# U's six transfers on ScalarE's queue, separate signals for U's lower parts, and K's maximum subtracted in two instructions

## What is computed

```python
def phi(x):                                   # 128 features, then both signs: 256
    proj = einsum('bhsd,df->bhsf', x, w_phi)
    proj = proj - max(abs(proj), axis=-1)
    return concatenate([exp(proj), exp(-proj)])
q_p, k_p = phi(q), phi(k)
kv  = einsum('bhsf,bhsd->bhfd', k_p, v);  z = sum(k_p, tokens)
x   = (q_p @ kv) / (q_p @ z + 1e-6)           # heads side by side: 576 x 512
h   = x.T @ U @ V;  u = x + h.T               # U: 576 x 32, V: 32 x 576
x2  = u + relu(u @ w_ch1) @ w_ch2             # 512 -> 2048 -> 512
h   = relu(x2.T @ w_tok1) @ w_tok2;  u = x2 + h.T
out = u + relu(u @ w2_ch1) @ w2_ch2           # 512 -> 1536 -> 512
```

## Time and profile before

| | us |
|---|---|
| median of 3 runs (lowest, highest) | 965.28 (965.09, 967.3) |
| profiled execution, its own time | 961.59 |
| its span | 959.6 |
| PE busy | 953.0, 99% |
| PE weight loads (PEld) | 828.7, 86% |
| DVE busy | 510.3, 53% |
| ACT busy | 373.4, 39% |
| POOL busy | 238.1, 25% |

### The profile page before, as it was taken

One profiled execution on the slowest core, in us unless ns is written; L12 is line 12 of the kernel. 1 busy time (PEld: TensorE's weight loads), 2 busy tenths in 40 slices (PEclk: granted clock), 3 DMA queues, 4 the chain that ended last, 5 costly groups with the idle time before them and its releaser, 6 DMA issues.

```text
span 959.6 us, 14152 instructions
## 1 busy us (share of the span) xinstructions
PE 953.0 (99%) x5398; PEld 828.7 (86%) x5398; DVE 510.3 (53%) x1005; ACT 373.4 (39%) x795; POOL 238.1 (25%) x148
## 2 busy tenths in 40 slices
PE   8999999999999999999999999999999999999998
PEld 7998888888888888888888889988888888888898
DVE  6756777667777658777542332433443343343232
ACT  6757667726675445665321112322202211111111
POOL 4357566704344214432120002530000000000000
PEclk9999999999999999999999999999999999999999
DMA  7651111111111011110052005532142132010010
GB/s 194 179 206 29 45 29 37 44 44 44 30 37 44 22 59 29 45 44 9 7 182 89 23 1 176 182 99 77 50 116 83 50 94 92 13 44 1 1 44 23
DMA packets 43043, 62.75 MB, mean 65 GB/s; under 512 B 10657, under 2 KB 30305, under 8 KB 41953
## 3 DMA queue, kind: packets, MB, share of 16 engines
q1 hardware_dynamic: 34752, 52.59, 18.0%
q10 hardware_dynamic: 8224, 9.26, 2.9%
HBM read 47.68 MB, written 14.16 MB: 64 GB/s over the span
## 4 chain that ended last, share of the span: by engine, by line
PE 97%; SPq 1%; DMA 1%; DVE 1%; issue 0%; ACT 0%; ACTq 0%; DVEq 0%
PE ps_ring L875 50%; PE ps_a L875 15%; PE ps_m L875 8%; PE ps_m L748 5%; PE ps_t L719 2%; PE ps_ring L757 1%; PE ps_a L775 1%; PE ps_a L770 1%; PE ps_a L769 1%; PE ps_a L710 1%; PE ps_t L732 1%; PE ps_t L661 1%; PE ps_t L660 1%; PE ps_t L659 1%; PE ps_m L743 1%; PE ps_a L788 1%
## 5 line engine op out<-in xcount | busy, mean ns | idle before, releaser
L875 PE MATMUL ps_ring<-u_hi,w_hi 128*128 128x512 f32 (+1 forms) x376 | 143.5, 382 | 0.1
L875 PE MATMUL ps_ring<-h_hi,w_hi 128*128 128x512 f32 (+1 forms) x376 | 143.0, 380 | 0.0
L875 PE MATMUL ps_ring<-u_hi,w_lo 128*128 128x512 f32 (+1 forms) x376 | 141.0, 375 | 0.0
L875 PE MATMUL ps_ring<-u_lo,w_hi 128*128 128x512 f32 (+1 forms) x376 | 140.9, 375 | 0.0
L875 PE MATMUL ps_ring<-h_lo,w_hi 128*128 128x512 f32 (+1 forms) x376 | 140.8, 374 | 0.0
L875 PE MATMUL ps_ring<-h_hi,w_lo 128*128 128x512 f32 (+1 forms) x376 | 140.5, 374 | 0.0
L1028 ACT ACTIVATE h_hi<-ps_ring 128x512 fp32r<-128x512 f32 (+1 forms) x94 | 53.1, 565 | 173.9 <-PE ps_ring L875 173.2
L1255 DVE SCALAR_TENSOR_TENSOR h_lo<-ps_ring,h_hi 128x512 fp32r<-128x512 f32 (+1 forms) x94 | 60.8, 649 | 106.6 <-ACT h_hi L1028 106.5
L1320 POOL TENSOR_TENSOR q_features_lo<-q_features_t,q_features_hi 128x576 fp32r<-128x576 f32 x48 | 67.7, 1432 | 116.9 <-ACT q_features_t L957 116.9
L1338 POOL TENSOR_TENSOR w_lo<-w_raw,w_hi 128x1024 fp32r<-128x1024 f32 x28 | 67.6, 2430 | 116.6 <-ACT w_hi L988 115.4
L875 PEld LDWEIGHTS ps_ring<-h_lo,w_hi 128*128 128x128 f32 x376 | 70.8, 188 | 13.4 <-DVE h_lo L1255 0.2
(11 more groups left out here) (218 smaller groups left out, 1948.2 us busy)
## 6 DMA issues: line engine op xcount, KB each, us to landing
w_raw<-in_wa SPq DMA_DIRECT2D x16, 512.0 KB, 5.0
w_raw<-in_wb SPq DMA_DIRECT2D x12, 512.0 KB, 3.9
v_one<-in_v_aug SPq DMA_DIRECT2D x28, 165.0 KB, 2.2
x_features<-x_scratch SPq DMA_DIRECT2D x4, 1152.0 KB, 5.9
x_by_tokens<-x_turned SPq DMA_DIRECT2D x16, 288.0 KB, 5.4
u_full<-x_scratch SPq DMA_DIRECT2D x4, 1152.0 KB, 5.1
kq_raw<-in_q_t SPq DMA_DIRECT2D x28, 160.0 KB, 2.9
x_tokens<-x_by_tokens SPq DMA_DIRECT2D x16, 256.0 KB, 2.7
```

The source lines that it names most:

```text
L875: last = pe.matmul(ps, w, x, start=(k, m) == (0, 0), stop=ended)
```

## The change

Four edits.

1. U's six transfers are taken out of SyncE's list and issued by ScalarE, two each ahead of `kv(0)`, `exp_k(1)` and `kv(1)` in its list: the four full tiles, the upper half, the lower half of the last.
2. `diff_last`, a new signal: in batch 0 VectorE subtracts the maximum in two instructions, first the last tile (128x128), then the four full ones (128x512). The exp of the last tile waits for the first, the other two for the second.
3. `xl_done` is raised by both instructions of VectorE's `pair_t`. `pair_l` waits for the first ahead of its first matmul and for the second ahead of its fifth. The other waits for `xl_done` count double.
4. `WARM[1]` is 5 for 3.

```diff
-WARM = 10, 3
+WARM = 10, 5
...
-            if n == 2:
-                for cols in (slice(0, RANK), slice(2 * RANK, P)):
-                    sp.dma_start(U4[:, 0:FULL, cols], u4[:, 0:FULL, cols]).then_inc(sem["u4_in"], 16)
-                    for rows in HALF:
-                        sp.dma_start(U4[rows, FULL, cols], u4[HALF[0], FULL, cols]).then_inc(sem["u4_in"], 16)
...
-                    pe.wait_ge(sem["xl_done"], (B - 1) * DT)
+                    pe.wait_ge(sem["xl_done"], 2 * (B - 1) * DT)
...
-            wait(pe, "xl_done", pairs - DT)
+            wait(pe, "xl_done", 2 * (pairs - DT))
...
-                pe.wait_ge(sem["xl_done"], pn - DT + 1)
+                pe.wait_ge(sem["xl_done"], 2 * (pn - DT) + 1)
                 for t in range(ST):
+                    if t == FULL:
+                        pe.wait_ge(sem["xl_done"], 2 * (pn - DT) + 2)
...
-                act.wait_ge(sem["diff_done"], n + 1)
+                act.wait_ge(sem["diff_last" if first else "diff_done"], n + 1)
...
                     act.activation(kp(n)[:, 2 * FULL], DIFF0[:, FULL], ACT.Exp, scale=SIGN[:])
+                    act.wait_ge(sem["diff_done"], n + 1)
...
+        def load_u4(rows, tiles, source):
+            for cols in (slice(0, RANK), slice(2 * RANK, P)):
+                act.dma_start(U4[rows, tiles, cols], u4[source, tiles, cols]).then_inc(sem["u4_in"], 16)
+
         for name, n in PROLOGUE["act"]:
+            if (name, n) == ("kv", 0):
+                load_u4(slice(0, P), slice(0, FULL), slice(0, P))
+            if (name, n) == ("exp_k", 1):
+                load_u4(HALF[0], FULL, HALF[0])
+            if (name, n) == ("kv", 1):
+                load_u4(HALF[1], FULL, HALF[0])
...
-                    dve.tensor_tensor(DIFF0[:], proj, MK[:, 0:ST].unsqueeze(2).to_broadcast([P, ST, DF]),
-                                      ALU.subtract).then_inc(sem["diff_done"], 1)
+
+                    for tiles, done in ((slice(FULL, ST), "diff_last"), (slice(0, FULL), "diff_done")):
+                        dve.tensor_tensor(DIFF0[:, tiles], proj[:, tiles], MK[:, tiles].unsqueeze(2).to_broadcast(
+                            [P, tiles.stop - tiles.start, DF]), ALU.subtract).then_inc(sem[done], 1)
...
-                                  XPH[:, 0:FULL].rearrange("p t f -> p (t f)").bitcast(F32), ALU.subtract)
+                                  XPH[:, 0:FULL].rearrange("p t f -> p (t f)").bitcast(F32), ALU.subtract).then_inc(sem["xl_done"], 1)
```

More of the change, by code:

```diff
@@ L502, in mixer_kernel @@
         rk_in_0 rk_in_1 rk_again_0 rk_again_1 rq_in_0 rq_in_1 v_in_0 v_in_1 k0_hi k0_lo k_split_hi k_split_lo q_split_hi q_split_lo
-        pk_done tsum_done mk_done diff_done kp_done pqt_done rq_done mt_done mrow_done mhi_done mlo_done mt_spread
+        pk_done tsum_done mk_done diff_last diff_done kp_done pqt_done rq_done mt_done mrow_done mhi_done mlo_done mt_spread
         pt_done qp_done qpl_done v_ones kv_done kv_copied kvl_done out_done den_turned den_done rden_done rden_rows x_done
```

## The result

The changed kernel takes **959.44 us** (959.08 to 960.68, 4 executions). Beside it, on the same chip, the kernel before took 966.29 us (965.09, 965.28, 967.3, 968.15). The ratio is 0.993, 95% interval 0.9908 to 0.9951, so 6.9 us less. The profiled execution took 959.12 us, its span is 957.1 (961.59 and 959.6 before). Between the two profiled executions the gain is thus only 2.5 us, close to the 2.8 of the forecast. The other 4.4 are the subject of this text.

The account below looks back on a forecast made before the run. TensorE, busy 953.0 of 959.6 us, was taken as the bound, with gains at kv(2) and the 12 pair_l steps: 0.80 + 1.98 = 2.8 us off the median 965.28 gave 962.5 us, range 960.4 to 965.5.

Parts of the forecast that it names:

- The step that failed: Final sum: the 2.8 us gain on the profiled execution was applied to the runs' median, 965.28, giving 962.5.
- The forecast's own upper bounds: Largest gains allowed: 0.95 us at kv(2) and 2.85 us at the pair_l steps.
- U's transfers off SyncE's queue: Head 4's K issued near 13.7 instead of 16.68, so kv(2) loses its wait; 0.80 us (0.55 to 0.95).
- The rival that the transfers are the bound: Head 4's K still lands at 21.9 and kv(2) stays; 963.3 us, chance 0.08.
- The six issues on ScalarE: U's issues in ScalarE's program, 1.2 to 1.7 us per two, covered by its idle times; cost taken as 0.
- The slower rival: ScalarE stands still while issuing, 1.64 us for each of six; 4.0 us slower, 969.3 us, chance 0.06.
- Two subtractions: Batch 0 on VectorE: 0.08 us more per head, four-tile exps 0.24 sooner; sum 0 within 0.1 outside kv(2).
- Warm-ups: Four added passes, some 0.5 us, fill part of the 0.8 us before turn_r(0); worth 0.
- The pairs: Two signals at pair_l: 0.27 us at three long sites, 0.13 at nine short ones; 1.98 us together.
- the first rival: The pairs give their gain back, as TensorE then waits for ScalarE or VectorE; 964.5 us, chance 0.12.
- the rival by which all the weight loads' idle time comes back: At pair_l all the idle time returns, 2.85 us, 3.7 us in all; 961.6 us, chance 0.14.
- What is released behind L811 starts from TensorE's ends and moves with them: Argument that work behind pair_l's product moves earlier with TensorE, so the pairs' gain is not given back.

Follow-up runs that it names:

- warm5_only: Kernel before with only the warm-up calls ahead of turn_r(0) raised from three to five; 963.01 us, ratio 0.9994.
- pairs_only: Kernel before with only the two signals for U's lower parts at pair_l; 964.89 us, ratio 0.9987.
- diff_only: Kernel before with only the subtraction split in two; 966.92 us, ratio 1.001.
- u_only: Kernel before with only U's six transfers moved to ScalarE's queue; 961.22 us, ratio 0.9957.
- u_later_sp: Kernel before with U's six transfers still on SyncE's queue, but behind head 4's K; 961.00 us, ratio 0.9959.
- u_diff: Kernel before with U's transfers on ScalarE's queue and the two subtractions; 960.89 us, ratio 0.9951.
- u_pairs: Kernel before with U's transfers on ScalarE's queue and the two signals for U's lower parts; 960.26 us, ratio 0.9946.
- after_warm3: Changed kernel with the warm-up calls ahead of turn_r(0) back at three; 959.61 us, ratio 0.9956.
- after_swap: Changed kernel with VectorE's turn_r(1) put ahead of its out(0); 959.46 us, ratio 0.9939.
- fill_kv2: Kernel before with four more calls of products on ones on TensorE ahead of kv(2); 962.35 us, ratio 0.9979.
- six_small_sp: Kernel before with U's transfers on ScalarE's queue and six 16-row by 8-column transfers at their old place on SyncE's; 961.85 us, ratio 0.9973.

## Why the prediction was wrong, point by point

**The step that failed** is one sentence: "the median of the runs, 965.28, lies 3.7 above, and the same gain there gives 962.5". It took the 3.7 us between the profiled execution and the median for a constant. It is not: it is what the fall of the clock costs in the executions that have one, and the change takes away what led to it. At clock 1.0 the kernel before takes 961.9 and the changed one 959.6, 2.3 less; the rest of the 5.8 to 6.9 us is that two thirds of the old executions were longer, most by 3 to 7 us, and none of the new ones is. The range failed by the same step: the scatter of the runs before, 965.09 to 967.3, was read as noise about a median. The profiled execution itself took 961.59; three executions of 965.09 or more beside it say that something in them is different which the one profile does not hold. (The forecast's own upper bounds, 0.95 and 2.85, add to 3.8, not 3.7; nothing hangs on it.)

How sure the cause is: with head 4's K late, the clock stood in 47 of 139 executions (before, warm5_only, pairs_only, diff_only); with K early in 83 of 87 (u_only, u_later_sp, u_diff, u_pairs, after_warm3, and the changed kernel and after_swap, 16 and 12); with K late and four calls run in the wait in 11 of 12. Both profiles that caught a fall show it inside the idle time at kv(2). That idle time there leads to the fall is shown. What decides it in a single execution is open, and the length of the idle time alone does not: there was no fall with 0.70 us at kv(2) (the profile before) nor with 0.98 (fill_kv2), one with 1.67 and one with 1.17, but that one came when only 0.4 us of it had passed; and none with 1.17 us ahead of turn_r(0) in u_only. Four executions in 87 fell with K early, one of them only to 0.998 and 961.37 us. No profile shows one of these, nor one of the twelve at 970 to 978 before; a late K of a later head, as in u_pairs, is a possible cause, not a shown one.

**U's transfers off SyncE's queue: right.** K of head 3 at 9.56 (9.6 foretold), of head 4 at 13.57 (13.7), its copy at 20.00 (20.23), kv(2) at 22.67 for 22.8 to 23.0, directly behind turn_r(2). It stands 1.03 sooner, for 0.80. The two traces must be read from the same place, though: kv(0) is already 0.16 sooner, and turn_r(0) lies anywhere from 9.27 (pairs_only) to 9.79 (diff_only), and at 10.85 in warm5_only. From kv(0) to kv(2) it is 14.05 us before, 13.24 in u_only and 13.18 in the changed kernel, so U's move is worth 0.81 there. The rival that the transfers are the bound is refuted by this, and six_small_sp shows the issues at work.

**The six issues on ScalarE: right, 0.** They took 0.39, 0.53, 0.47, 0.61 and 1.12 for two, 3.1 us for 3.6 to 5.0 foretold, and run beside its casts and exps: the copy (L919) starts at 9.62 while the first issue lasts until 9.67. v_k's copy is at 11.72. The slower rival is gone with it.

**Two subtractions: right in mechanism.** From the first's start to the block maximum it is 0.81 (20.81 to 21.62) for 0.74 before, 0.07 more, so the second is not held, as by the rule of the Trainium skill (VectorE: DVE Perf Modes, Two Vector instructions with no wait between them). The forecast put their worth at 0 outside kv(2). From head 0's first subtraction to kv(0) it is 1.85 us in u_diff and 1.93 in u_only and before, and from kv(0) to kv(3) 21.12 for 21.25: 0.2 us in all, of which 0.06 falls between kv(0) and kv(2). The 0.41 between the two kernels' times has scatter in it; u_diff is already 0.35 ahead at turn_r(0).

**Warm-ups: right, 0.**

**The pairs: 1.98 foretold, 1.33 measured**, and here the first rival was half right. The lead of the changed kernel over the one before, read at equal instructions of the two traces, is 1.13 us ahead of the first pair (101 us) and 2.46 behind the last (474 us), and stays there to the end. At the sites themselves it rises by 0.13 to 0.16 at the nine short ones and 0.29 to 0.30 at the three long ones, 2.2 in all, more than foretold, though less than the 2.85 of the rival by which all the weight loads' idle time comes back. But 0.8 to 0.9 of this is given back within some us. Behind the fourth pair (long) and the eighth (long), PEld before, then after:

```profile
201.40 0.19 PEld L829 LDWEIGHTS ps_ring<-v_split,xu 128*128 128x128 f32 x1
...
334.72 0.19 PEld L875 LDWEIGHTS ps_ring<-h_hi,w_hi 128*128 128x128 f32 x1 [0.27 <-DVE acc L1190]
```

```profile
199.88 0.19 PEld L826 LDWEIGHTS ps_ring<-v_split,xu 128*128 128x128 f32 x1 [0.35 <-issue]
...
332.66 0.19 PEld L872 LDWEIGHTS ps_ring<-h_hi,w_hi 128*128 128x128 f32 x1 [0.51 <-DVE acc L1200]
```

At the eighth pair TensorE is 2.38 us ahead at pair_l, but VectorE's sum into `acc` is only 2.06 ahead (333.98 and 331.92), because its chain starts from the casts of x, not from pair_l; TensorE waits 0.51 for it instead of 0.27, and is 2.09 ahead behind it. At the fourth it is the same chain on VectorE, 1.52 ahead (its sum into `acc` at 200.28 and 198.76), behind which the lower part of `xu` is made. Two long sites are thus worth nothing net. Three short ones keep next to nothing as well: behind the third and the eleventh pair the weight loads of proj_k (L705) wait 0.37 us for 0.20 and 0.19, and behind the tenth 0.37 for 0.33, after 0.21 for VectorE's sum into `u_full`. "What is released behind L811 starts from TensorE's ends and moves with them" was wrong for these five. The sixth pair, foretold at 276.3, is at 276.16.

## What to carry to other kernels

Before a gain read from one profiled execution is carried over to a median, ask why the two differ, and look at the granted clock of every execution; a gap of 3.7 us with a profile at full clock is a term of its own. An idle time of TensorE of one or two microseconds, in which little is lost by the list of waits, cost 4 to 5 more behind it here: remove it, or, if that cannot be done, try products that nobody reads in part of it. And a wait removed in one engine's list is worth what the next wait leaves of it, so follow the lead from instruction to instruction, not site by site.

## What the hardware showed that was not expected

- The granted clock fell to half (0.50, 1.2 GHz) inside an idle time of 1.17 and one of 1.67 us, after 0.4 and 1.6 us of it, in a kernel whose TensorE was busy otherwise. It rose again after about 10.2 us in both, TensorE being busy without a gap since the idle time. From kv(2) to kv(3) that cost 4.5 and 4.8 us, and whole executions with a fall mostly took 965.0 to 968.9 us for 961.9.
- Whether it fell differed from execution to execution of the same kernel: 68 of 103 before.
- The same transfer, head 4's K, in the same place of the queue's list, was issued at 16.68, 16.54, 18.24 and 17.01 us in four profiles, and its copy started at 22.01, 22.85, 23.45 and 23.61.
- Six transfers of 16 rows by 8 columns took SyncE 2.76 us to issue, nearly as long as U's six (3.5 us). Single issues took up to 2.42 us (head 6's K in u_pairs) where the same one took 0.66 in the changed kernel.
- In warm5_only ten passes of the warm-up took 2.06 us, 1.31 in the changed kernel, with the granted clock given as 1.00 in both: the profile's clock does not show the slower pace of the first 10 us.
